# Second products of two token chunks in seven block products, their low parts made on GpSimd

## The reference

```python
def _moe2_ref(x, w_in, w_out):      # w_in 512 x 2048, w_out 2048 x 512
    h = x @ w_in
    g = h * np.cos(h)
    return (g @ w_out).astype(np.float32)
```

## Time and profile before

| | |
|---|---|
| median of 3 runs | 811.18 us (811.05 to 812.61) |
| profiled execution | 811.25 us, its span 809.5 us |
| PE busy | 802.3 us (99%), 4404 matmuls |
| DVE busy | 581.0 us (72%) |
| ACT busy | 291.9 us (36%) |
| POOL busy | 227.9 us (28%), none of it after 555 us |
| granted TensorE clock | 1.000 throughout (the upper of the two levels, 2.4 GHz) |

### The profile page before, as it was taken

The page is one execution under the profiler, slowest core; times in us unless marked ns, Lnnn a source line. Parts: engine busy times, 40 slices in busy tenths (PEclk is TensorE's granted clock), DMA queues, the critical chain, the costliest instruction groups (busy, mean ns, idle before and its releaser), DMA issues.

```text
span 809.5 us, 11379 instructions
## 1 busy us (share of the span) xinstructions
PE 802.3 (99%) x4404; PEld 677.6 (84%) x4404; DVE 581.0 (72%) x962; ACT 291.9 (36%) x548; POOL 227.9 (28%) x230
## 2 busy tenths in 40 slices
PE   8999999999999999999999999999999999999998
PEld 7888888888888888888888888888888888888886
DVE  6887766766766767767667658577777787777766
ACT  4743222222222222322222322246454554545442
POOL 3976343334333333433433433242000000000000
PEclk9999999999999999999999999999999999999999
DMA  8941100120110111101011011000011001100004
GB/s 326 334 151 56 50 27 27 40 78 27 40 38 27 40 66 40 40 27 40 28 39 40 27 39 40 27 27 28 26 40 40 27 27 40 39 27 28 1 0 156
DMA packets 19865, 44.83 MB, mean 55 GB/s; under 512 B 2344, under 2 KB 2392, under 8 KB 19812
## 3 DMA queue, kind: packets, MB, share of 16 engines
q1 hardware_dynamic: 19812, 44.10, 16.6%
HBM read 40.93 MB, written 3.17 MB: 54 GB/s over the span
## 4 chain that ended last, share of the span: by engine, by line
PE 97%; DMA 1%; POOL 1%; DVE 1%; SPq 0%; ACT 0%; issue 0%
PE ps L1020 33%; PE ps L1001 28%; PE ps L1082 16%; PE ps L1101 16%; PE ps L968 1%; PE ps L918 1%; DMA att<-att_in 1%; PE ps L932 1%; PE ps L955 1%; POOL h_lo L440 1%; PE ps L942 1%; DVE att L661 0%; SPq L288 0%; DVE temps L795 0%; DVE y L865 0%; DVE temps L753 0%
## 5 line engine op out<-in xcount | busy, mean ns | idle before, releaser
L440 POOL TENSOR_TENSOR h_lo<-temps,h_hi 128x512 fp32r<-128x512 f32 (+1 forms) x128 | 135.3, 1058 | 295.3 <-ACT h_hi L540 295.2
L540 ACT ACTIVATE h_hi<-temps 128x512 fp32r<-128x512 f32 (+1 forms) x128 | 67.3, 526 | 336.9 <-DVE temps L758 336.9
L741 DVE TENSOR_TENSOR y<-ps,y 128x512 f32<-128x512 f32 x180 | 124.0, 689 | 71.8 <-PE ps L1020 71.8
L1020 PE MATMUL ps<-h_hi,w_hi 128*128 128x512 f32 x384 | 150.5, 392 | 0.1
L1001 PE MATMUL ps<-x_hi,w_hi 128*128 128x512 f32 (+1 forms) x448 | 150.4, 336 | 0.1
L1001 PE MATMUL ps<-x_hi,w_lo 128*128 128x512 f32 (+1 forms) x448 | 150.5, 336 | 0.0
L1001 PE MATMUL ps<-x_lo,w_hi 128*128 128x512 f32 (+1 forms) x448 | 150.5, 336 | 0.0
L1020 PE MATMUL ps<-h_lo,w_hi 128*128 128x512 f32 x384 | 150.3, 391 | 0.0
L1020 PE MATMUL ps<-h_hi,w_lo 128*128 128x512 f32 x384 | 149.4, 389 | 0.0
L1001 PEld LDWEIGHTS ps<-x_hi,w_hi 128*128 128x128 f32 x448 | 84.7, 189 | 12.8 <-DVE temps L772 0.3
L1001 PEld LDWEIGHTS ps<-x_lo,w_hi 128*128 128x128 f32 x448 | 84.7, 189 | 11.7
(11 more groups left out here) (84 smaller groups left out, 1113.3 us busy)
## 6 DMA issues: line engine op xcount, KB each, us to landing
w_raw<-w_in SPq DMA_DIRECT2D x96, 256.0 KB, 2.6
att<-att_in SPq DMA_DIRECT2D x24, 512.0 KB, 7.0
temps<-p_scr SPq DMA_DIRECT2D x4, 768.0 KB, 4.0
out<-y SPq DMA_DIRECT2D x12, 256.0 KB, 2.0
att<-dp_in SPq DMA_DIRECT2D x1, 24.0 KB
p_scr<-att SPq DMA_DIRECT2D x1, 24.0 KB
lam<-lam_in SPq DMA_DIRECT2D x1, 6.0 KB, 1.6
```

Of the source, the lines that this page charges most:

```text
L440: pool.tensor_tensor(hs_lo[side][:, f, at], ring(s, i), f32(hs_hi[side][:, f, at]), ALU.subtract).then_inc(s_hlo, 1)
L540: act.activation(hs_hi[s % SIDES][:, f, at], ring(s, i), ACT.Copy).then_inc(s_hhi, 1)
L741: dve.tensor_tensor(at, from_bank, at, ALU.add).then_inc(s_y, 1)
L1020: mm = pe.matmul(ps[:, DOWN_BANK + g % DOWN_BANKS, :], ww[:, s // SIDES % 2, f, at], hh[side][:, f, tokens], start=(f == 0 and n == 0), st ...
```

## The change

In the quarters 0 to 6 of the MLP, the second products of chunks 0 and 1 are taken together. With the two blocks f, the two halves of the output columns (256 each) and the two chunks they are a 2x2 by 2x2 block product, and seven block products take the place of eight. A block product is two tiles of 3 matmuls (groups 0 to 13 of a quarter, two for each row of `SECOND`). Chunk 2 keeps its four tiles of 6 matmuls (groups 14 to 17); two of these (15 and 17) stay in banks 6 and 7 over the quarters. The seven results are summed over the quarters in seven areas of 128x1024, and seven additions (`combined`) in the last quarter put them together. The last quarter has 12 groups of 6 matmuls, as before.

Four sums of gates are made on DVE in each quarter (`token_sum`, t2[0] to t2[3]) and four sums of weights on GpSimd (`w2_sums`). All low parts in the MLP are made on GpSimd (`token_low`, `w_low`, `w2_sums_low`): nine of tokens, four of weight pieces and one of 128x1024. There are now 3 banks for up products (`UP_BANKS`), 3 that the other groups share in turn (`SECOND_BANKS`), and 2 kept ones. `MIX` says after which quarter of an up product a group stands: slot v - 4 = 6 m + t, t from 0 to 5.

```diff
-LAG = 4
-GATE_BANKS = 4
+UP_BANKS = 3
+SECOND = (((0, 0), 0, (None, 0)), ((1, 0), 1, (0, 0)), ((None, 0), 3, (1, 1)), ((None, 3), 2, (0, 1)),
+          ((None, 2), 5, (None, 2)), ((None, 1), 4, (None, 1)), ((1, 256), 6, (1, 0)))
+SPLITS = (0, 1, 3, 2, 5, 4, 6, 7, 8)
+MIX = (((0,), (1,), (2,), (3,)), ((), (4,), (), (5,)), ((6,), (7,), (8,), (9,)), ((10,), (11,), (12,), (13,)),
+       ((14,), (), (15,), ()), ((16,), (), (17,), ()))
+MIX_LAST = tuple(((), (2 * t,), (), (2 * t + 1,)) for t in range(6))
+SECOND_BANK, SECOND_BANKS, KEPT_BANK = 3, 3, 6
...
+            pool.wait_ge(s_wlo, w2_count(QUARTERS, 1))
+            for m in range(FULL):
+                q = QUARTERS + m
+                w2_sums(m)
+                gate_low(m, 0, 0)
+                w1_low(q + 1, 0)
+                gate_low(m, 1, 1)
+                w2_sums_low(m)
+                token_low(m, 2, t2[0])
+                w1_low(q + 1, 1)
+                gate_low(m, 3, 3)
+                token_low(m, 4, t2[1])
+                token_low(m, 5, t2[2])
+                token_low(m, 6, t2[3])
+                gate_low(m, 7, 4)
+                w2_low(q + 1, 0)
+                gate_low(m, 8, 5)
+                w2_low(q + 1, 1)
...
+                elif j == 3:
+                    sum_high(m, 2, 0)
+                elif j == 4:
+                    gate_high(m, 3, 3)
+                    sum_high(m, 4, 1)
+                elif j == 5:
+                    gate_high(m, 7, 4)
                 act.wait_ge(s_r2, v + 1)
...
+                    if j == 2:
+                        w2_sums_high(m)
+                    if j == 4:
+                        sum_high(m, 5, 2)
+                        sum_high(m, 6, 3)
...
-                down2(2 * (v - LAG))
+                second(v, 3)
                 dve.wait_ge(s_r1, v + 1)
                 dve.scalar_tensor_tensor(out=rr[:, t, :], in0=kf[:, t, :], scalar=-C2, in1=rr[:, t, :],
                                          op0=ALU.mult, op1=ALU.add).then_inc(s_r2, 1)
-                if v >= 1:
-                    gate_low(v - 1)
-                down2(2 * (v - LAG) + 1)
...
+                if m < FULL and j == 4:
+                    token_sum(m, 3, 3, t2[3], gate_of(m, 1), t2[2])
+                second(v + 1, 0)
...
                 dve.scalar_tensor_tensor(out=gg[:, t, :], in0=cs[:, t, :], scalar=1.0, in1=bank, op0=ALU.subtract,
                                          op1=ALU.mult).then_inc(s_gate, 1)
...
+                if m < FULL and j == 2:
+                    dve.wait_ge(s_gate, 6 * m + 3)
+                    token_sum(m, 0, 0, t2[0], gate_of(m, 2), gate_of(m, 0))
+                if m < FULL and j == 3:
+                    dve.wait_ge(s_gate, 6 * m + 4)
+                    token_sum(m, 1, 0, t2[1], gate_of(m, 3), gate_of(m, 2))
+                    token_sum(m, 2, 1, t2[2], gate_of(m, 3), t2[0])
...
+                second(v + 1, 1)
+                second(v + 1, 2)
...
+                        r = rotating(m, i)
+                        bank = ps[:, SECOND_BANK + r % SECOND_BANKS, :]
+                        if r >= SECOND_BANKS:
+                            pe.wait_ge(s_y2, r - SECOND_BANKS + 1)
...
+            for v in range(GATES + 4):
+                for part in range(KT):
+                    if v < GATES:
+                        up2(v, part)
+                    second(v, part)
```

More of the change, by code:

```diff
@@ L457, in _ @@
+            for j in range(6):
+                gate_low(FULL, j, j)
         @block.scalar
@@ new lines, in gate_of, with token_sum, combined @@
+            def gate_of(m, j):
+                return gg[:, (6 * m + j) % T_RING, :]
+            def token_sum(m, i, after, at, one, other):
+                if m:
+                    dve.wait_ge(s_glo, split_done(m - 1, (2, 4, 5, 6)[i]))
+                if after:
+                    dve.wait_ge(s_t2, 4 * m + after)
+                dve.tensor_tensor(at, one, other, ALU.subtract).then_inc(s_t2, 1)
+            def combined(n, at, one, other):
+                if n:
+                    dve.wait_ge(s_comb, n)
+                dve.tensor_tensor(at, one, other, ALU.add).then_inc(s_comb, 1)
@@ L1105, in _ @@
-            for v in range(GATES):
-                for part in range(2):
-                    up2(v, part)
-                    down2(2 * (v - LAG) + part)
+                    if v >= UP_BANKS:
+                        pe.wait_ge(s_gate, v - UP_BANKS + 1)
+                of = slice(512 * f + P * part, 512 * f + P * (part + 1))
+                for n, (ww, xx) in enumerate(((w1_hi, x2_hi), (w1_hi, x2_lo), (w1_lo, x2_hi))):
+                    mm = pe.matmul(ps[:, v % UP_BANKS, :], ww[q % 2][:, of], xx[:, part, chunk(c)],
+                                   start=(part == 0 and n == 0), stop=(part == KT - 1 and n == 2))
@@ new lines, in up2, with second_tile, halves @@
+                if part == KT - 1:
+                    mm.then_inc(s_g, 1)
+            def second_tile(bank, pieces, opens, closes):
+                for n, (w, x) in enumerate(pieces):
+                    mm = pe.matmul(bank, w, x, start=(opens and n == 0), stop=(closes and n == len(pieces) - 1),
+                                   skip_group_check=True)
+                mm.then_inc(s_dn2, 1)
+            def halves(q, f, d, row):
+                at = slice(P * d, P * (d + 1))
+                hi, lo = w2_hi[:, q % 2, f, at], w2_lo[:, q % 2, f, at]
+                return [(hi, h2_hi[:, row, :]), (hi, h2_lo[:, row, :]), (lo, h2_hi[:, row, :])]
```

275 lines of the change are left out of this document (196 added, 79 removed).

## The result

The kernel became slower: 847.93 us (846.89 to 849.6, 4 runs) against 811.89 us (811.05 to 814.7, 4 runs), a ratio of 1.0445 with an interval of [1.0426, 1.0464]. The direction was forecast, the size was not: the time lies 5 us above the range (806 to 843) and above the likeliest case's own (819 to 845). The profiled execution took 849.6 us, its span 846.3 us.

The account below looks back on a forecast made before the run. It took PE's matmuls, 0.227 us each, to bound the kernel. 811.25 - 9.5 (fewer matmuls) - 0.3 (bank 3) + 23.1 (seven quarters) + 3.1 (start) + 2.8 (end) = 830.4, said as 830 us; range 806 to 843.

Parts of the forecast that it names:

- the likeliest case: Whole kernel: DVE's chain over gates plus waits for the port shared with GpSimd makes PE wait; 819 to 845 us, chance 0.59.
- The chain without port waits: Steady quarter: PE reaches group 10 at 15.44 us, group 7's bank is free at 16.40; PE waits 1.0 us a quarter.
- The port waits by place: Steady quarter: r2 and sums of gates wait for GpSimd's instruction; +0.3, +0.9, +0.2, two of 0 or about 1, 0 to +0.7.
- PE stays the bound: Rival: no steady wait of PE is left after the change; about 805 us, faster; chance 0.17.
- r2 isn't caught: Rival: the chain without port waits, r2 with its int32 operand not held by GpSimd; 814.4 us, range 808 to 819; chance 0.18.
- I take 3.3, with one of the two ties lost: Steady quarter: loss of 3.3 us chosen from 2.3 to 5.0; over seven quarters +23.1 us.
- the two ties: Near-simultaneous requests with GpSimd's low parts: t2[2] against gate 3's (0 or +1.1), r2 of gate 5 against gate 4's (0 or +1.0).
- behind group 10: Steady quarter: r2 of the next gate 0 can meet a low part, and group 14 needs group 11's bank; 0 to +0.7 us.
- The chain itself: Steady quarter: DVE and ACT steps from k of gate 3 to group 7, ended at 16.40 us before port waits.
- 38 instructions for 40, no load to speak of: DVE's quarter: loses 10 low parts, gets 4 sums and 4 more groups, so no added load was counted.
- The start: Start of the MLP: group 0 waits for gate 0's low part behind GpSimd's queue; +3.1 us, at least 1.
- The end: Last quarter: the seven `combined` additions (8.0 us) make DVE late and group banks free late; +2.8 us, bounds 0 and 5.

Follow-up runs that it names:

- narrow: Kernel after, with every GpSimd instruction of the MLP cut to 16 columns, order and semaphores unchanged: 816.0 us, 1.0055 against the kernel before.
- r_psum: Kernel after, with r1's result written to a PSUM bank from gate 6 on, four banks in turn for groups, none kept: 817.04 us, 1.0061 against the kernel before.
- evac_first: Kernel after, with groups 1 and 2 taken out of their banks ahead of the sums t2[1] and t2[2]: 844.99 us, 1.0396 against the kernel before.
- banks5: Kernel after, with five banks in turn for the groups instead of three and two kept ones: 847.31 us, 1.0432 against the kernel before.
- k_first: Kernel after, with ScalarE's k of gate 5 ahead of two high parts and a weight piece: 842.02 us, 1.0367 against the kernel before.
- best2: Kernel after with r_psum, evac_first and k_first, three final additions on GpSimd, low parts of the first two and last two gates on VectorE: 807.22 us.
- best1: Kernel after with r_psum, evac_first and k_first, first weight sums ahead of x's low parts, three final additions on GpSimd: 810.45 us.

## Why the prediction was wrong in size

**Right.** 4362 matmuls. The chain without port waits: 1.0 us a quarter forecast, 1.1 in narrow. The port waits by place: +0.9 at r2 of gate 3 (measured 1.56 - 0.68 = 0.88), +0.2 at t2[1] (0.88 - 0.70), +1.0 at r2 of gate 2 (1.67); which instructions are caught and which aren't (L1077 at 1.31 us against "near 1.0", L1095 and L1044 at 0.69 and 0.68). One wait of 3.3 us for L563 at the start, forecast 3.1. k of gate 5 is over 2 us late. The rule of the Trainium skill ("SBUF — State Buffer", section "SBUF: two separate sides"), that the port is locked for a whole instruction, agrees with the rows: the caught instructions end 0.55 us behind GpSimd's. The rivals that PE stays the bound and that r2 isn't caught fell with the profile after. What the second would have cost is shown by narrow and r_psum, where r2 isn't caught: 816 and 817 us, and it was given 814.4.

**The step that failed** is the steady quarter's "I take 3.3, with one of the two ties lost". It measured 5.08, at the upper bound of 5.0 (the terms as listed add up to 2.4 and 5.2, not to 2.3 and 5.0). Both ties were lost: t2[2] has a mean of 1.76 us over six quarters, and r2 of gate 5 takes 1.64. They aren't coin tosses: the same order of instructions returns each quarter and gives the same result. That is about 1.05 us a quarter more. The other 0.6 us is behind group 10: the wait at group 14 (0 to 0.7 forecast) is 0.44, and PE's restarts, 0.11 us each, I hadn't counted at all.

The chain itself held. From k of gate 2 to k of gate 3 it gave 5.74 us, and 5.73 were measured (700.88 to 706.61). From there to group 7's tile it gives 15.71 + 0.9 + 0.2 and the two ties, 1.1 + 1.0, which makes 18.9; 18.76 were measured (706.61 to 725.37). From group 14 to group 10 PE needs 30.31 us for 114 matmuls (695.79 to 726.10), a loss of 4.5 us, and the terms up to there, with both ties lost, are 1.0 + 0.3 + 0.9 + 0.2 + 2.1 = 4.5. The places were half wrong: groups 7 to 10 lose 2.3 us as forecast, but 2.0 us stand at group 4 already, where "hardly" any had been forecast. evac_first shows that these are one lateness, as it reappears at group 7. The catching up in the slots 1 and 2 was right too: k of gate 2 waits 0.90 us for PE in every quarter.

What was left out is a second limit close behind. "38 instructions for 40, no load to speak of" counts instructions and not DVE's time. Its round is 29.0 us of work, of which r2's port waits are 6 x 0.63 = 3.8 and those of the sums 1.3, and 4.6 us of waiting for squares: 33.6 against PE's 31.28. So with these port waits, the removal of waits for banks and for k can't give back more than 2.7 of the 5.08, and banks5 and k_first gave back 0.77 and 0.74. The 2.6 us that DVE waits for k are 1.33 at gate 2 (where k waits for PE), 0.53 at gate 3 and 0.75 at gate 5; only the last was tested. The 4.6 us for the squares, which more instructions between r2 and the gate had all but filled before, weren't tested at all: an order that fills them again, with everything else as in the kernel after, is the rival remedy that no run tried.

**The start**, +3.1, was right for the wait and missed what follows: the low clock behind it (1.7 us with the restart), and a first quarter that loses 3.8 instead of 3.3 us. **The end**, +2.8 with bounds 0 and 5, was 6.3. Group 7's wait was forecast as 1.5 us and is 1.60 (836.04). Two things weren't in the sum: group 3 waits 2.13 us, and 1.7 us go to matmuls at the lower clock behind it. Timeline of the kernel after, two of the `combined` and PE's wait for a bank:

```profile
822.23 1.54 POOL L563 TENSOR_TENSOR x_lo<-temps,x_hi 128x512 fp32r<-128x512 f32 x1 [3.34 <-ACT x_hi L740]
822.66 3.46 DVE L1061 TENSOR_TENSOR y<-y,h_f 128x1024 f32<-128x1024 f32 x2
...
826.97 0.50 PE L1302 MATMUL ps<-x_hi,w_hi 128*128 128x512 f32 x1 [2.13 <-DVE y L1037]
```

The additions themselves were priced at 8.0 us in all, without the port: here two take 3.46 us instead of 2.4. DVE doesn't come into the last quarter late: the k of its gates 2 and 3 wait 1.43 and 0.73 us for PE (809.91 and 815.35). In best2 three additions are on GpSimd, two low parts on VectorE, and each group waits for its own addition; a single wait of 0.46 us is left there. The term was not tested by itself.

## What to carry to other kernels

When work is moved to an idle engine, look for the instructions of the relieved engine that the newcomer will catch, and price them along the chain from one wait to the next. Where two engines meet in a repeated order, each tie falls the same way every time, so take it as lost in all rounds or in none, and give both prices. Then add up the whole round of the relieved engine too, with the stretching by the shared port and the waits for dependent steps that the new order leaves open, and compare it with the bound: it says how little the removal of single waits can give back. The cheap remedy here was to let the caught instruction read one operand from PSUM: that single operand was worth 30 us, several times what reordering gave, and only then were the saved matmuls worth anything.

## What the runs showed of the hardware

- A scalar_tensor_tensor with an int32 and a float32 operand, both in SBUF, waits for GpSimd as a tensor_tensor does: 1.31 us on average against 0.68 with one operand in PSUM. It ends 0.55 us behind GpSimd's instruction.
- GpSimd is held up too, but less: the low part on t2[0] takes 1.77 us instead of 1.29.
- A wait of PE costs more than its length. The first matmul behind it starts 0.33 us ahead of the next instead of 0.23, and the clock can fall. Busy time of two stretches in the kernel after, behind waits of 3.3 and 2.1 us (columns as above):

```profile
561.00:565.20 4.20, 4.20 (x12) 3.25 (x12) 3.02 (x6) 2.29 (x5) 4.20 (x3) 0.59 0.49 185
828.00:831.40 3.40, 3.40 (x9) 2.31 (x7) 2.04 (x5) 2.36 (x4) 0.00 (x0) 0.50 0.35 131
```

The granted clock is 0.59 and 0.50, the lower of the two levels (1.2 GHz) for most of them, and matmuls start 0.43 us apart. Behind the 1.7 us at group 4 of each quarter it stayed at 1.00, as it did behind the 2.1 us at 564.20 in best2, while it fell to 0.52 behind 1.77 us in best1. What decides it isn't shown by these runs.
